# Fused mixing and two products on one core: weight pieces loaded in two halves, taps for 64 channels on TensorE, and low weights finished by adding transfers

## The reference

```python
w = softmax over the 7 taps of weight            # 8 heads x 7 taps, head = channel // 24
x[b, s, d] = sum over k of w[head(d), k] * x_pad[b, s + k, d]     # 6 zeros ahead of each sequence
x = x.reshape(8192, 192)
h = x @ w_in_1;  g = h * sigmoid(h);                  x = g @ w_out_1     # layer one, 2048 wide
h = x @ w_in_2;  g = where(h > 0, h, exp(min(h, 0)) - 1);  out = g @ w_out_2      # layer two
```

## Time and profile before

| what | us |
|---|---|
| median of 3 runs | 1127.65 (1127.58 to 1127.73) |
| the profiled execution | 1127.64 |
| its span (first to last instruction) | 1125.8 |
| PE busy | 1117.3 (99% of the span) |
| DVE busy | 779.1 (69%) |
| ACT busy | 640.6 (57%) |
| POOL busy | 0.3 |

### The profile page before, as it was taken

One profiled execution on the slowest core, in us unless ns is written; L12 is line 12 of the kernel. 1 busy time (PEld: TensorE's weight loads), 2 busy tenths in 40 slices (PEclk: granted clock), 3 DMA queues, 4 the chain that ended last, 5 costly groups with the idle time before them and its releaser, 6 DMA issues.

```text
span 1125.8 us, 22725 instructions
## 1 busy us (share of the span) xinstructions
PE 1117.3 (99%) x9728; PEld 1104.9 (98%) x9728; DVE 779.1 (69%) x951; ACT 640.6 (57%) x732; POOL 0.3 (0%) x5
## 2 busy tenths in 40 slices
PE   9999999999999999999999999999999999999998
PEld 6899999999999999999999999999999999999997
DVE  8766578888755636888875553787886654387776
ACT  6566665555556655545555565545466555555553
POOL 0000000000000000000000000000000000000000
PEclk9999999999999999999999999999999999999999
DMA  4301100001000000000100000000011000000000
GB/s 144 110 16 32 51 1 1 15 15 29 11 20 15 15 1 1 10 6 15 30 17 14 15 16 1 1 15 7 10 29 29 1 1 1 1 1 15 15 1 29
DMA packets 17394, 21.48 MB, mean 19 GB/s; under 512 B 1936, under 2 KB 12176, under 8 KB 17296
## 3 DMA queue, kind: packets, MB, share of 16 engines
q1 hardware_dynamic: 17152, 20.03, 6.3%
q10 hardware_dynamic: 144, 0.01, 0.0%
HBM read 13.74 MB, written 6.29 MB: 18 GB/s over the span
## 4 chain that ended last, share of the span: by engine, by line
PE 98%; DVE 1%; ACT 1%; issue 0%; DVEq 0%
PE acc L617 50%; PE hid L601 46%; PE acc L726 1%; DVE glo L457 0%; PE acc L718 0%; PE acc L721 0%; DVE mixb L363 0%; ACT g L329 0%; PE acc L601 0%; PE acc L720 0%; ACT ghi L325 0%; ACT x L272 0%; DVE wi L402 0%; DVE mixa L363 0%; DVE ghi L444 0%
## 5 line engine op out<-in xcount | busy, mean ns | idle before, releaser
L601 PE MATMUL hid<-x,wi 64*128 64x512 f32 x4335 | 690.1, 387 | 0.4
L601 PEld LDWEIGHTS hid<-x,wi 64*128 64x128 f32 x4335 | 561.1, 184 | 5.5 <-PE acc L601 2.3
L617 PE MATMUL acc<-ghi,wo 64*128 64x512 f32 x3036 | 540.5, 387 | 0.2 <-DVE ghi L444 0.2
L457 DVE TENSOR_TENSOR glo<-g,ghi 128x1024 fp32r<-128x1024 f32 x256 | 313.6, 1225 | 320.6 <-ACT g L329 179.7
L617 PE MATMUL acc<-glo,wo 64*128 64x512 f32 x2024 | 425.6, 387 | 2.4 <-issue 2.2
L617 PEld LDWEIGHTS acc<-ghi,wo 64*128 64x128 f32 x3036 | 415.2, 184 | 1.6 <-issue 0.6
L617 PEld LDWEIGHTS acc<-glo,wo 64*128 64x128 f32 x2024 | 300.9, 184 | 3.9 <-issue 2.6
L329 ACT ACTIVATE g<-hid 128x1024 f32<-128x1024 f32 x255 | 261.4, 1025 | 29.3 <-PE hid L601 29.2
L297 ACT ACTIVATE ghi<-g 128x1024 fp32r<-128x1024 f32 x128 | 135.8, 1061 | 231.6 <-DVE g L465 231.6
L325 ACT ACTIVATE ghi<-hid 128x1024 fp32r<-128x1024 f32 x126 | 129.6, 1029 | 205.0 <-PE hid L601 205.0
L465 DVE SCALAR_TENSOR_TENSOR g<-hid,g 128x1024 f32<-128x1024 f32 x128 | 156.7, 1224 | 4.4
(11 more groups left out here) (56 smaller groups left out, 226.0 us busy)
## 6 DMA issues: line engine op xcount, KB each, us to landing
xa<-x_rows SPq DMA_DIRECT2D x16, 259.0 KB, 2.9
stg<-w_in SPq DMA_DIRECT2D x16, 256.0 KB, 3.2
outT<-stg SPq DMA_DIRECT2D x16, 256.0 KB, 2.0
stg<-w_out SPq DMA_DIRECT2D x16, 192.0 KB, 3.2
xb<-x_rows SPq DMA_DIRECT2D x32, 65.5 KB, 2.7
outT<-tail SPq DMA_DIRECT2D x16, 128.0 KB, 2.3
tap<-tap_rows ACTq DMA_DIRECT2D x1, 7.0 KB, 3.0
```

Of the source, the lines that this page charges most:

```text
L457: eng.tensor_tensor(glo[:, u % NG, :], g[:, u % 2, :], ghi[:, u % NG, :].bitcast(F32), ALU.subtract).then_inc(s_glo, 1)
L601: return eng.matmul(hidden_part(u, t), wt, mv, start=t == home and n == 0, stop=t == home and n == 4 if 0 < u < LAG else t != home and n == 3)
L617: return eng.matmul(acc[s % 2][:, bank, :], wt[rows, 2 * j + t, cols], mv, start=leads and j == 0 and n == 0, stop=not leads and j == NPAI ...
```

## The change

Seven things are edited together.

1. Staging: w_in and w_out of a piece are loaded, waited for and released apart (`load_in`, `load_out`; semaphores `s_stgi`, `s_stgo`, `s_wih`, `s_woh` in place of `s_stg`, `s_whi`). SP's order at the start is chunk zero, w_in 0, 1, 2, w_out 0, w_in 3, w_out 1 to 3, chunk one; later pieces go out w_in first, each when its slot's w_in is split.
2. The narrow taps of chunk zero move from VectorE to TensorE. POOL makes an identity, ScalarE makes seven diagonal matrices of tap weights, TensorE multiplies them in full fp32 with the shifted input and sums in PSUM, ScalarE copies the sum to `mixb`. The warm-up is 9 products ahead and 6 behind.
3. ScalarE's order at the start: exponentials, diagonals, three w_in splits, copy of the mix, one narrow conversion, the wide one, three narrow ones, then the table for the activation (before: ahead of all splits), w_in 3, w_out 0.
4. `begin` has three row waits and four stretches (3, 8, 12 and 4 pairs) in place of five row waits ahead of its last part.
5. Unit 1's gate is now also rounded by VectorE (`round_gate`), so ScalarE runs one activation for it.
6. For units 3 to 6 of layer one, VectorE no longer makes the low w_out. ScalarE writes minus the high part (two copies with scale -1), and two DMAs from POOL's queue add the weights to it in SBUF. The second product of these units waits for the adds. (In the kernel's list of 16 pieces, these are the numbers 3 to 6 of `ADDED`.)
7. Chunk one: its second narrow tap moves one period later, and both its low parts go in front of unit 6's residue.

```diff
-            return [2, 2, 3, 3, 3, 4, 4, 4, 4, 5, 5, 5, 5, 5][i]
+            return [2, 2, 3, 3, 3, 4, 4, 4, 5, 5, 5, 5, 5, 5][i]
...
+    ADDED = (3, 4, 5, 6)
     def piece_period(q):
-        return q - 2 if q < NPAIR else SPLIT2[q - NPAIR]
+        if q >= NPAIR:
+            return SPLIT2[q - NPAIR]
+        return q - 2 if q > NSTG else 1
+    def out_period(q):
+        if q >= NPAIR:
+            return SPLIT2[q - NPAIR]
+        return q - 1 if q < 7 else 7
-    ROWS0, ROWS = 6, 5
-    WARM = 30
+    ROWS0, ROWS = 3, 5
+    WARM = (9, 6)
...
+        ident = g[:, 0, 0:P]
+        diag = [g[:, 1, i * P:(i + 1) * P] for i in range(NTAP)]
+        mix0 = acc[0][:, 1, 0:HT]
...
+            todo = [(-30 if c == 0 else -10 if c == 1 else -1 if c == 2 else tap_period(c - 2, 1, NTAP - 1) + 0.5,
+                     0, load_x, c) for c in range(NCHUNK)]
+            todo += [([-29, -28, -27, -25][q] if q < NSTG else -8 + q if q < 7 else 0.3 if q == 7 else
+                      piece_period(q - NSTG) + 0.3, 1, load_in, q) for q in range(NPIECE)]
+            todo += [([-26, -24, -23, -22][q] if q < NSTG else -1.5 if q == NSTG else
+                      out_period(q - NSTG) + 0.4, 1, load_out, q) for q in range(NPIECE)]
...
         @block.gpsimd
+            eng.memset(ident, 1.0).then_inc(s_ident, 1)
+            eng.wait_ge(s_ident, 1)
+            eng.affine_select(ident, ident, [[-1, P]], ALU.is_equal, 0.0, base=0, channel_multiplier=1)\
+               .then_inc(s_ident, 1)
+            for i, q in enumerate(ADDED):
+                l, j = divmod(q, NPAIR)
+                wt = wo[l][:, 2 * j:2 * j + 2, :]
+                eng.wait_ge(s_neg, adds_before(q + 1))
+                eng.dma_start(wt[:, :, D + REST:2 * D], out_rows(q)[:, :, 0:P], accum_op=ALU.add).then_inc(s_add[i], 16)
+                eng.dma_start(wt[:, :, D:D + REST], out_rows(q)[:, :, P:D], accum_op=ALU.add).then_inc(s_add[i], 16)
...
+            def hi_out(q):
+                l, j = divmod(q, NPAIR)
+                wt = wo[l][:, 2 * j:2 * j + 2, :]
+                eng.wait_ge(s_stgo[q % NSTG], 16 * (q // NSTG + 1))
+                eng.activation(wt[:, :, 0:D], stg_out(q), ACT.Copy).then_inc(s_woh, 1)
+                if q in ADDED:
+                    eng.activation(wt[:, :, D + REST:2 * D], stg_out(q)[:, :, 0:P], ACT.Copy, scale=-1.0)\
+                       .then_inc(s_neg, 1)
+                    eng.activation(wt[:, :, D:D + REST], stg_out(q)[:, :, P:D], ACT.Copy, scale=-1.0)\
+                       .then_inc(s_neg, 1)
...
+            eng.wait_ge(s_exp, 2)
+            eng.wait_ge(s_ident, 2)
+            for i in range(NTAP):
+                eng.activation(diag[i], ident, ACT.Copy, scale=tap[:, 1, i:i + 1]).then_inc(s_diag, 1)
+            for q in range(3):
+                hi_in(q)
+            eng.wait_ge(s_mix0, 1)
+            eng.activation(mixb[:, :], mix0, ACT.Copy).then_inc(s_tapb, NTAP)
+            eng.wait_ge(s_tap, 5)
+            conv_hi_b(0, 0)
+            conv_hi_a(0)
+            for part in range(1, 4):
+                conv_hi_b(0, part)
             eng.wait_ge(s_tab, 2)
             eng.activation(tstat[:, 6:7], tstat[:, 7:8], ACT.Silu).then_inc(s_tab, 1)
-            split_hi(0)
-            split_hi(1)
-            eng.wait_ge(s_tap, 5)
-            conv_hi_a(0)
-            split_hi(2)
-            split_hi(3)
-            conv_hi_b(0, 0)
-            conv_hi_b(0, 1)
+            hi_in(3)
+            hi_out(0)
...
+                if c == 0:
+                    q = l * NPAIR + j
+                    eng.wait_ge(s_woh, q + 1)
+                    if q in ADDED:
+                        eng.wait_ge(s_add[ADDED.index(q)], 32)
+                    else:
+                        eng.wait_ge(s_wol, lows_before(q + 1))
...
             def begin():
+                for n in (2, 3):
+                    if n == 3:
+                        eng.wait_ge(s_chib, 4)
+                        eng.wait_ge(s_xlo, 3)
+                    half_first(0, LOW, 1, n)
+                    last = half_first(0, HIGH, 0, n)
                 last.then_inc(s_row, 1)
                 eng.wait_ge(s_row, 2)
+                for u in range(LAG):
+                    for n in range(1, 5):
+                        half_first(u, LOW, 0, n)
+                        last = half_first(u, HIGH, 1, n)
...
+            warm(WARM[0])
+            eng.wait_ge(s_xb[0], 32)
+            for i in range(NTAP):
+                eng.wait_ge(s_diag, i + 1)
+                last = eng.matmul(mix0, diag[i], xb[:, 0, i:i + HT], start=i == 0, stop=i == NTAP - 1)
+            last.then_inc(s_mix0, 1)
+            warm(WARM[1])
             begin()
```

More of the change, by code:

```diff
@@ L85, in low_b_period, with lows_before, adds_before @@
         return NPAIR * stage_of(c, 0) - (3 if c % GROUP == 0 else 2)
+    ADDED = (3, 4, 5, 6)
     SPLIT2 = [15, 23, 24, 25, 27, 29, 30, 31]
     def piece_period(q):
-        return q - 2 if q < NPAIR else SPLIT2[q - NPAIR]
-    def piece_out_period(q):
-        return q if q < NPAIR else SPLIT2[q - NPAIR]
-    ROWS0, ROWS = 6, 5
-    WARM = 30
+        if q >= NPAIR:
[5 more added lines that the diff above has]
+        return q - 1 if q < 7 else 7
+    def lows_before(q):
+        return 2 * sum(1 for i in range(q) if i not in ADDED)
+    def adds_before(q):
+        return 2 * sum(1 for i in range(q) if i in ADDED)
+    ROWS0, ROWS = 3, 5
+    WARM = (9, 6)
     ctx = ExitStack()
@@ L170, in mixed_two_layer_ffn @@
         s_store = sem("s_store")
-        s_stg = [sem(f"s_stg{i}") for i in range(NSTG)]
-        s_whi = sem("s_whi")
+        s_stgi = [sem(f"s_stgi{i}") for i in range(NSTG)]
+        s_stgo = [sem(f"s_stgo{i}") for i in range(NSTG)]
+        s_wih = sem("s_wih")
+        s_woh = sem("s_woh")
+        s_neg = sem("s_neg")
+        s_add = [sem(f"s_add{i}") for i in range(len(ADDED))]
         s_wim = sem("s_wim")
@@ L179, in mixed_two_layer_ffn @@
         s_exp = sem("s_exp")
+        s_ident = sem("s_ident")
+        s_diag = sem("s_diag")
+        s_mix0 = sem("s_mix0")
         def stg_in(q):
@@ L267, in conv_hi_a, with conv_hi_b @@
                 eng.activation(x_of(0, c)[:, 0, :], mixa[:, :], ACT.Copy, scale=tstat[:, 4:5]).then_inc(s_chia, 1)
-            def conv_hi_b(c, half):
+            def conv_hi_b(c, part):
+                to, rows, at = [(LOW, LOW, 0), (HIGH, HIGH, HT), (HIGH, LOW, 0), (LOW, HIGH, HT)][part]
                 eng.wait_ge(s_tapb, NTAP * (c + 1))
-                for to, rows, at in [[(LOW, LOW, 0), (HIGH, HIGH, HT)], [(HIGH, LOW, 0), (LOW, HIGH, HT)]][half]:
-                    eng.activation(rest_hi(0, c, to)[:, at:at + HT], mixb[rows, :], ACT.Copy,
-                                   scale=tstat[rows, 5:6]).then_inc(s_chib, 1)
+                eng.activation(rest_hi(0, c, to)[:, at:at + HT], mixb[rows, :], ACT.Copy,
+                               scale=tstat[rows, 5:6]).then_inc(s_chib, 1)
             def swap_rest(s):
@@ L321, in _ @@
                     eng.wait_ge(s_hid, u + 1)
-                    if layer(u // NPAIR) == 0 and u:
+                    if layer(u // NPAIR) == 0 and u >= 2:
                         if u >= NG:
@@ L329, in _ @@
                     eng.activation(g[:, u % 2, :], hidden(u), fn).then_inc(s_fn, 1)
-                for q in range(NSTG, NPIECE):
-                    if piece_period(q) == u:
-                        split_hi(q)
+                for q in range(1, NPIECE):
+                    if q >= NSTG and piece_period(q) == u:
+                        hi_in(q)
+                    if q < 7 and out_period(q) == u or q >= 7 and out_period(q) == u:
+                        hi_out(q)
                 for s in range(NSTAGE):
@@ L342, in _ @@
                         conv_hi_a(c)
-                    for half in range(2):
-                        if hi_b_period(c, half) == u:
-                            conv_hi_b(c, half)
+                    for part in range(4):
+                        if hi_b_period(c, part // 2) == u:
+                            conv_hi_b(c, part)
         @block.vector
@@ L531, in _ @@
                                 conv_tap(c, grp, k)
-                    if low_a_period(c) == u:
+                    if c > 1 and low_a_period(c) == u:
                         conv_low_a(c)
-                    if low_b_period(c) == u:
+                    if c > 1 and low_b_period(c) == u:
                         conv_low_b(c)
@@ L601, in half_first @@
                 return eng.matmul(hidden_part(u, t), wt, mv, start=t == home and n == 0,
-                                  stop=t == home and n == 4 if 0 < u < LAG else t != home and n == 3)
+                                  stop=t == home and n == 4 if u == 0 else t != home and n == 3)
             def half_second(u, rows, bank, n):
@@ L662, in begin @@
                 last.then_inc(s_row, 1)
-                eng.wait_ge(s_row, 6)
+                eng.wait_ge(s_row, 3)
                 for u in range(1, LAG):
```

(13 more changed lines are left out.)

122 lines of the change are left out of this document (50 added, 72 removed).

## The result

The changed kernel takes 1121.2 us in the median of 5 runs (1121.12 to 1121.95) against 1127.65 for the kernel before: ratio 0.9949, 95% interval 0.9938 to 0.9959. Forecast were 1121.7 and a range of 1120.5 to 1124.3. The profiled execution took 1121.14, with a span of 1119.4 against 1125.8. The marker, ScalarE's start on unit 8's hidden block, moved from 51.05 to 44.64: 6.41, and the span shrank by 6.4. So everything was decided ahead of 60 us, as the prediction had it.

A forecast was written before the change was run, and what follows sets the result against it. It took the bound to be work ahead of 60 us, up to ScalarE's start on unit 8: 4.3 from TensorE going on earlier plus 1.65 of clock, 5.95, taken from 1127.64 gives 1121.7 us; range 1120.5 to 1124.3.

The forecast's parts named there:

- The sum: Marker before unit 8: 4.3 us from TensorE going on at 41.4 instead of 45.69, plus 1.65 of clock, 5.95.
- TensorE's mixing: At the start: diagonals 0.40 each, products 0.43 at the high level, mix ready at 9.3, first product at 11.1.
- the low end that was given: At the start: VectorE's wide taps bind, not the mix, and TensorE's first product stays at 10.64.
- The first three units: TensorE's start: six stretches become four, each drain costs 0.35, gate 0 is there at 16.55.
- VectorE's chain: Gate 0 to chunk one's last narrow tap takes 22.6, ending at 39.2; four low w_out, 2.1, are gone.
- The clock: After TensorE's stop in unit 8, cut from 2.2 to 0.6: no fall of the level, so 1.65 comes back.
- The mix late: Rival at the start: low TensorE level or slow diagonals shift VectorE's chain by up to 2.3: 1124.0; chance 0.13.
- The clock falling again: Rival in unit 8: the clock falls even after the shorter stop, costing 1.65: 1123.4; chance 0.12.
- The adds in series: Rival in units 3 to 6: adds go one after another; at 8.6 each, 12.6 late: 1134.3; chance 0.06.
- VectorE held up by POOL: Rival: each of POOL's eight transfers costs VectorE 0.5, so 4.0 is lost: 1125.7; chance 0.08.
- The change not shortening the start: Rival: something on ScalarE, late identity or table load, gives back as much: 1126 to 1128; chance 0.06.
- Loads: SP's sixteen pieces, w_in and w_out apart: nothing late, cost nothing; tightest is unit 5's low w_in, some 0.5 ahead.

The follow-up runs named there:

- no adds: Changed kernel with no adding transfers, so VectorE makes all low w_out again: 1123.64 us.
- six stretches: Changed kernel with the first three units on TensorE in the old six stretches instead of four: 1123.67 us.
- the two with clears: Changed kernel with two, then four idle clears on VectorE ahead of chunk one's low parts: 1122.14 and 1123.53 us.
- four clears: Changed kernel with four idle clears on VectorE ahead of chunk one's low parts: 1123.53 us.
- 20 warm-ups: Changed kernel with 20 warm-up products ahead of the mix in place of 9: 1123.84 us.
- unit 2 added: Changed kernel with unit 2's low w_out also made by adding transfers and its w_in split moved behind the wide conversion: 1121.52 us.
- adds only: Kernel before with only the adding transfers, their negated copies and the waits for them: 1124.17 us.

## Why the prediction was right

**The sum.** Marker 44.64 against 45.1 forecast, TensorE going on at 40.90 against 41.4, time 1121.2 against 1121.7. Of the 0.5, 0.45 is one term.

**TensorE's mixing: the term that was mis-sized.** "First product at 11.1" was 10.65, the low end that was given: VectorE's wide taps ended last (9.84), not the mix. Seven diagonals took 2.16, 0.31 each against 0.40, so the three splits ended at 8.54 instead of 9.4. The mix ended at 8.64 against 9.3: a product cost 0.47 against 0.43, but TensorE's rows were fast from the mix's start on, not only from 6.7. (The warm-up's row gives 3.55 / 8 = 0.44 a product, not 0.43; on nine products that is 0.1.) The low end is in part luck of this execution. In four kernels whose start is the same (no adds, six stretches, the two with clears) the first product came at 10.78 to 11.16, because the third w_in split waited 0.16 to 0.82 for its load, and with four clears because the mix ended at 9.03; there ScalarE's queue binds, as the prediction had it. The products go by the four partial products that were assumed; the Trainium skill (FP8 and Floating Point Precision, section TensorE Precision Notes) says that true FP32 makes four passes, and the 0.45 measured with 20 warm-ups is that.

**The first three units.** 4.4 from the first product to gate 0 was forecast, 4.43 measured, drains of 0.35 included (the second stretch again began 1.03 after the first). The table load and its dummy ended at 13.7, the splits behind them at 14.65: 0.43 ahead of gate 0, the thin cover held.

**VectorE's chain.** From the rounding of gate 0 to the last tap 22.6 was forecast, 38.71 - 16.14 = 22.57 measured; ScalarE's four narrow conversions 2.1, measured 38.74 to 40.85. The four low w_out that went were priced at 2.1; the kernel without adds gives 2.02.

**The clock.** No fall was the right call, and stops of 0.26, 0.69 and 1.58 show it. The argument rested on the nearest rows, 0.35 and 2.2; the runs with VectorE delayed show that the stop and not something else near it makes the difference. What the prediction did not see is that before's 1.65 is not in every execution: against those of its runs without it (some 1126.2) the gain is 5.0, not 6.45. The forecast took it from one profiled execution that has it, and the median has it too because four of the five runs of before beside the changed kernel do, to judge by their times. That is in part luck: over all later runs it is 20 of 38, and beside the 20 warm-ups before's median was 1126.88.

**The rivals.** The mix late: not in the profiled execution, but in a mild form in others. TensorE's rows became fast later in the execution with unit 2 added (a mix of 4.09, first product at 11.38), and the third w_in split waited for its load in the four kernels named above; the start now passes on such delays in full, as the 20 warm-ups show, and this is the likely reason for the changed kernel's own spread of 0.8, though its other executions were not profiled. The clock falling again: not at this stop. The adds in series: they landed 4.0 and 5.4 us after issue (medians; the latest 5.8), against 4.3 taken; the second of a pair goes out 0.85 behind the first, and none is late. VectorE held up by POOL: its residues have a mean of 1223 ns, 1221 before; no 4 us. The change not shortening the start: refuted by 2.67. The Trainium skill (SBUF — State Buffer, section Who interferes with whom) lets VectorE's tensor_scalar operations collide with GpSimd's, and here the traces agree only in part: the first wide tap, 0.48 before, took 0.73 beside a POOL issue with unit 2 added and 0.70 in the kernel with adds only, but 0.50 in the changed kernel and 0.48 to 0.51 in four others, where a POOL issue ran beside it as well. It is at most 0.25 us of VectorE.

**Loads.** "Cost nothing" held in the profiled execution of the changed kernel. In kernels with the same start the third w_in came late, by up to 0.82, and held up the first product. What staging in halves is worth by itself is not shown.

## What to carry to other kernels

Find the one moment behind which nothing can move, and do the sum to it along the engine that is late, start to start: terms of 22.6, 4.4 and 2.1 us came out within 0.1. Two repairs of one stall do not add up when the stall has an all-or-nothing consequence: each alone saves the clock, so undoing one shows only the rest. When work is moved off the engine that is late, see how close the engine that takes it over comes: here ScalarE drew level, and the next relief gave nothing. And look at the runs one by one before pricing such a term: a median can hold a cost that part of the executions do not pay.

## What was not expected of the hardware

- **A stop and the lower level.** In the kernel whose profiled stop is 1.77 the granted clock fell to 0.50 (1.2 of 2.4 GHz), and three of seven runs have the lower mean clock; with 2.18 it is 20 of 38, with 1.58 none of five. The level did not fall during the stop: TensorE went on at 42.61, and it was still 1.00 from 43.0 to 43.5 and 0.50 from 44.0.
- **The first microseconds.** The granted clock reads 1.00 from 1.5 us on, yet the warm-up's rows show half pace: 0.42 us for each of nine 512-column products (0.47 in four other kernels), where a pair of 512-column matmuls on the two halves takes 0.227 later. At what moment they become fast differs between executions: behind the same nine products the mix, from 5.53 on, took 3.26 without the adds and 4.09 with unit 2 added.
- **Adding transfers.** POOL's row for the issue of a 128 KB transfer is 1.2 to 1.3 us long and 1.7 for one of 64 KB, which also lands later (5.4 against 4.0). The rows of a pair overlap: the second starts 0.73 to 0.85 behind the first.
- **Weight loads.** PEld busy from 60 to 100 us fell from 40.00 to 33.04 at an unchanged period of 4.31 us a unit (ScalarE starts on unit 8 at 44.64 and on unit 9 at 48.95), so it is worth no time. It is not the change that does it: with four clears the changed kernel shows 40.00 too. Why it differs is open.
